# Attention loads in another order on the DMA queue, a term-by-term order for one matrix product, and weight halves split between its groups

## The reference

```python
def _attn_ref(q, k, v, beta):            # (4, 8, 768, 48)
    k_n = k / (np.linalg.norm(k, axis=-1, keepdims=True) + 1e-06)
    for t in range(S):
        kt, vt, bt = (k_n[:, :, t], v[:, :, t], beta[:, :, t, None])
        y[:, :, t] = np.einsum('bhd,bhde->bhe', q[:, :, t], state)
        v_old = np.einsum('bhde,bhd->bhe', state, kt)
        state = state + bt[:, :, :, None] * np.einsum('bhd,bhe->bhde', kt, vt - v_old)
...
def _moe_ref(x, w_ch1, w_ch2):           # x (4, 768, 384), w_ch1 (384, 1536), w_ch2 (1536, 384)
    X = np.fft.fft(x, axis=1)
    X = np.fft.fft(X, axis=2)
    u = x + np.real(X)
    un = (u - mu) / np.sqrt(var + 1e-06)
    return u + np.maximum(un @ w_ch1, 0.0) @ w_ch2
...
def _moe2_ref(x, w_in, w_spatial, b_spatial, w_out):   # the gated block, not changed
```

## Time and profile before

| | us |
|---|---|
| median of 3 runs | 889.29 |
| lowest, highest | 888.91, 891.04 |
| time of the profiled execution | 889.29 |
| its span, first to last instruction | 887.5 |
| PE busy | 822.8 |
| DVE busy | 473.3 |
| ACT busy | 294.3 |
| POOL busy | 197.8 |

### The profile page before, as it was taken

How to read it: one execution, slowest core, us unless ns; L and a number is a source line. 1 busy time by engine, 2 the same in 40 slices (tenths; PEclk the granted TensorE clock), 3 DMA queues, 4 the chain that set the end, 5 groups by cost and what they waited for, 6 DMA issues and landing times.

```text
span 887.5 us, 24710 instructions
## 1 busy us (share of the span) xinstructions
PE 822.8 (93%) x10634; PEld 797.0 (90%) x10634; DVE 473.3 (53%) x1072; ACT 294.3 (33%) x656; POOL 197.8 (22%) x171
## 2 busy tenths in 40 slices
PE   7378999899886999999999999999999999999998
PEld 6377899888776999999999999999899899899898
DVE  4999999999278743443434443333732431431421
ACT  5235566656343121112211221122531431421412
POOL 2123123034005605300720000000222222222321
PEclk9658989889996999999999999999999999999999
DMA  6544445412572120111002003003410010000001
GB/s 196 147 132 125 139 131 155 118 57 80 164 248 96 59 68 18 53 51 40 18 18 71 0 18 119 18 18 112 144 54 31 23 53 35 18 0 36 19 1 54
DMA packets 38170, 65.14 MB, mean 73 GB/s; under 512 B 4345, under 2 KB 26178, under 8 KB 38082
## 3 DMA queue, kind: packets, MB, share of 16 engines
q1 hardware_dynamic: 38082, 63.85, 23.2%
HBM read 46.66 MB, written 14.16 MB: 69 GB/s over the span
## 4 chain that ended last, share of the span: by engine, by line
PE 62%; issue 21%; DVE 13%; POOL 2%; ACT 2%; DMA 1%; SPq 0%; POOLq 0%; DVEq 0%; ACTq 0%
PE m_ps_h L1189 12%; PE g_ps_v L1690 11%; PE m_ps_d L1174 11%; PE ps_ga L449 4%; PE g_ps_y L1690 3%; PE g_ps_u L1690 3%; DVE prod L619 3%; PE ps_r L500 3%; DVE t_lane L623 2%; PE ps_y L540 2%; PE ps_y L535 2%; PE ps_u L518 2%; PE ps_s L553 2%; POOL g_vn_lo L1587 2%; PE ps_ga L474 2%
## 5 line engine op out<-in xcount | busy, mean ns | idle before, releaser
L1374 DVE SCALAR_TENSOR_TENSOR m_h_lo<-m_ps_h,m_h_hi 128x512 fp32r<-128x512 f32 x72 | 49.7, 691 | 101.7 <-ACT m_h_hi L1051 101.7
L1174 PE MATMUL m_ps_d<-m_w_hi,m_h_hi 128*128 128x384 f32 x288 | 97.6, 339 | 0.0
L1174 PE MATMUL m_ps_d<-m_w_hi,m_h_lo 128*128 128x384 f32 x288 | 96.3, 335 | 0.0
L1174 PE MATMUL m_ps_d<-m_w_lo,m_h_hi 128*128 128x384 f32 x288 | 96.3, 334 | 0.0
L1051 ACT ACTIVATE m_h_hi<-m_ps_h 128x512 fp32r<-128x512 f32 x72 | 43.1, 598 | 151.7 <-PE m_ps_h L1189 151.5
L449 PE MATMUL ps_ga<-kq 64*64 64x64 f32 x1536 | 61.0, 236 | 19.0 <-DVE t_lane L623 12.4
L1189 PE MATMUL m_ps_h<-m_unt_hi,m_w_hi 128*128 128x256 f32 x432 | 75.3, 283 | 3.4 <-DVE m_h_lo L1374 2.4
L449 PEld LDWEIGHTS ps_ga<-kq 64*64 64x64 f32 x1536 | 57.3, 150 | 19.9 <-DVE t_lane L623 12.6
L1189 PE MATMUL m_ps_h<-m_unt_hi,m_w_lo 128*128 128x256 f32 x432 | 74.3, 281 | 0.0
L1189 PE MATMUL m_ps_h<-m_unt_lo,m_w_hi 128*128 128x256 f32 x432 | 74.2, 281 | 0.0
L619 DVE TENSOR_TENSOR prod<-g_lane,t_lane 128x31 f32<-128x31 f32 (+15 forms) x186 | 69.6, 374 | 6.2
(11 more groups left out here) (223 smaller groups left out, 1920.7 us busy)
## 6 DMA issues: line engine op xcount, KB each, us to landing
kq<-kq_g SPq DMA_DIRECT2D x48, 256.0 KB, 3.3
v_in<-v_g SPq DMA_DIRECT2D x12, 384.0 KB, 3.3
k_in<-k_g SPq DMA_DIRECT2D x12, 384.0 KB, 3.1
x_scr<-y_sb SPq DMA_DIRECT2D x24, 192.0 KB, 3.5
stage<-w_ch SPq DMA_DIRECT2D x6, 768.0 KB, 5.7
x_scr<-m_x_sb SPq DMA_DIRECT2D x24, 192.0 KB, 1.9
g_x<-x_scr SPq DMA_DIRECT2D x24, 192.0 KB, 4.5
out<-g_y SPq DMA_DIRECT2D x24, 192.0 KB, 1.9
```

What stands on the lines that cost most here:

```text
L1174: last = pe.matmul(out, first[x], second[y], start=(k == 0 and m == 0), stop=(k == n - 1 and m == 2))
L1374: dve.scalar_tensor_tensor(h_lo[:, 2 * g:2 * g + 2].rearrange("p f t -> p (f t)"), ps_h[g % 2][:, :], 0.0, h_hi[:, 2 * g:2 * g + 2].rearra ...
```

## The change

Three edits, and no instruction is added or taken away on PE, DVE, ACT or POOL.

1. The SP list of the attention steps is written in another order. The wait on y_ok inside a step is gone. The last two quarters of a group's second kq half move from places 6 and 7 to places 0 and 1 of the next group, the second half of v from place 2 to place 1, and the store `results(g, 0)` ahead of the loads of place 7.
2. `hidden` waits for t_lo before its first product, and takes the 9 products of a tile through `three`: the three terms of one slice d after each other.
3. The low halves of chunks 3 and 4 move into the first `hidden`: DVE does chunk 3 after the group 0, chunk 4 after group 2, chunk 5 after group 4.

```diff
                 if k and k <= STEPS - NB:
                     sp.wait_ge(u_ok, k)
+                if n == N - 1 and g + 1 < G:
+                    results(g, 0)
                 if g and n < NB - 1:
                     results(g - 1, n + 1)
...
-                if 2 <= k <= STEPS - NB:
-                    sp.wait_ge(y_ok, k - 1)
...
+                if n < 2 and g + 2 < G:
+                    for p in ((2 + n,) if g else (2 * n, 2 * n + 1)):
+                        load_kq(g + 2, 1, p)
...
+                if 2 <= n < 6 and g + 3 < G:
+                    if g and n == 2:
+                        sp.wait_ge(y_done, N * g)
+                    load_kq(g + 3, 0, n - 2)
...
+                if n >= 6 and g + 3 < G:
+                    load_kq(g + 3, 1, n - 6)
...
-                pe.wait_ge(t_hi, b * R + (r + 1))
+                pe.wait_ge(t_lo, b * R + (r + 1))
...
-                            if f == 0 and m == 2:
-                                pe.wait_ge(t_lo, b * R + (r + 1))
...
+                        for d in range(DT):
+                            last = three(ps_h[g % 2][:, C2 * (f % 2):C2 * (f % 2) + C2],
...
-                    if first and g == 2:
-                        weights(WC - 1)
+                    if first and g % 2 == 0:
+                        weights(DT + g // 2)
...
-            weights(DT, NS)
             batch(0, True, False)
```

More of the change, by code:

```diff
@@ L221, in sync @@
                 g, n = k // N, k % N
-                two, three = g + 2 < G, g + 3 < G
                 if k and k <= STEPS - NB:
                     sp.wait_ge(u_ok, k)
+                if n == N - 1 and g + 1 < G:
+                    results(g, 0)
                 if g and n < NB - 1:
                     results(g - 1, n + 1)
-                if n == (1 if g else 0) and two:
+                if n == (1 if g else 0) and g + 2 < G:
                     diagonal(g + 2)
[L229 to L241, removed]
-                if 2 <= k <= STEPS - NB:
-                    sp.wait_ge(y_ok, k - 1)
-                if n in (0, 2) and g + 1 < G:
+                if n < 2 and g + 2 < G:
+                    for p in ((2 + n,) if g else (2 * n, 2 * n + 1)):
+                        load_kq(g + 2, 1, p)
+                if n < 2 and g + 1 < G:
                     if g and n == 0:
                         sp.wait_ge(preset_ok, p_count(N * g - 1) - 1)
-                    load_v(g + 1, n // 2)
+                    load_v(g + 1, n)
+                if 2 <= n < 6 and g + 3 < G:
+                    if g and n == 2:
+                        sp.wait_ge(y_done, N * g)
+                    load_kq(g + 3, 0, n - 2)
                 if n in (3, 5) and g + 1 < G:
@@ L1184, in hidden @@
                     for f in (2 * g, 2 * g + 1):
-                        for m, (w, t) in enumerate(((w1_hi, unt_hi), (w1_lo, unt_hi), (w1_hi, unt_lo))):
-                            if f == 0 and m == 2:
-                                pe.wait_ge(t_lo, b * R + (r + 1))
-                            for d in range(DT):
-                                last = pe.matmul(ps_h[g % 2][:, C2 * (f % 2):C2 * (f % 2) + C2],
-                                                 w[:, d, P * f:P * f + P], t[:, d], start=(m == 0 and d == 0),
-                                                 stop=(m == 2 and d == DT - 1))
+                        for d in range(DT):
+                            last = three(ps_h[g % 2][:, C2 * (f % 2):C2 * (f % 2) + C2],
+                                         [w[:, d, P * f:P * f + P] for w in (w1_hi, w1_lo)],
+                                         [t[:, d] for t in (unt_hi, unt_lo)], d, DT)
                     last.then_inc(h_done, 1)
```

## The result

| | before | after |
|---|---|---|
| runs on the same chip | 20 | 20 |
| median, us | 889.87 | 894.60 |
| lowest, highest | 885.21, 899.02 | 890.12, 901.16 |
| mean | 890.12 | 894.89 |
| profiled execution, us | 889.29 | 894.69 |

The forecast was 890.4, within 0.3% of no change. A second comparison of the same two kernels gave +4.1, give or take 1.1, so the loss is real. The single executions of one kernel scatter by about 3 us either way, and what follows has to live with that. The means count every run; in each series of the kernel before at most one run lies over 1.5% above its fastest and counts as slow, and without it the differences would be up to 0.5 us higher.

A forecast was written before the change was run, and what follows sets the result against it. PE was taken as the bound, by its own pace in the mixer and by instruction arrival in the attention. 889.29 + 0.7 (attention) + 0 (hidden pace) + 0.4 (first hidden) gave 890.4 us, range 886.6 to 895.0.

The forecast's parts named there:

- The first hidden: Mixer's first hidden: group 2 starts 0.9 us earlier, group 3 waits 2.4 us through POOL's port; +0.4 us at `result`.
- The bound and the stretches: Whole kernel: PE's own pace bounds the mixer after its first 26 us; the attention has 15.2 us of instruction-issue holes.
- The pace of the nine products: Hidden stages: term-by-term order leaves each at its pace, 113.3 or 117.8 ns a product; 0 us.
- The second rival: Hidden stages: term-by-term order may make all of them slow, +2.4 us, 892.8 us with the other terms; chance 0.12.
- the third: All hidden stages at 113.3 ns, 3.4 us less, or instruction packets relieved, 2.8 us less; 886.5 us, chance 0.12.
- Edit 1 as data: Attention: the removed waits guard no data and no load comes so late that PE must wait; costs nothing.
- Edit 1 as company of instruction packets: Attention: denser transfers in places 0 and 1 hold PE's instruction packets longer; +0.9 us, between 5.6 gained and 9 lost.
- the price of a meeting: Attention: an instruction packet beside heavy traffic holds its engine 1.86 instead of 0.99 us, at most 0.87 us more.
- Well over 19: Attention, 84 to 250 us: PE's issue waits should sum to 14 to 18 us; well over 19 would mean the first rival.
- the first rival: Attention: dense transfers in places 0 and 1 delay most instruction packets of the coupling products; 894 us, chance 0.20.
- The wait on t_lo: Start of hidden: PE starts 1.05 us later in the first one; 0 in the other 11.
- DVE caught again by POOL and its tokens late: Behind the first hidden: if POOL holds up both DVE operations again, tokens come 1.1 us later and the term is +1.2.

The follow-up runs named there:

- dense: The kernel before with all kq and k loads of a group at place 1, v loads at place 0, no y_ok wait: +2.4 ± 0.8 us, ratio 1.0040.
- calm: The kernel before with all kq, k and v loads of groups 1 to 3 at places 2 to 6, no y_ok wait: -2.5 ± 0.6 us, ratio 0.9983.
- the repeat: The whole change measured a second time against the kernel before: +4.1 ± 1.1 us, ratio 1.0048.
- null: The kernel before with the three slices d of hidden taken in falling order, all else the same: +0.2 ± 1.0 us, ratio 1.0016.
- the second look at edit 1: The SP list of the change alone, measured a second time against the kernel before: +2.4 ± 1.1 us, ratio 1.0030.
- few bytes: The kernel before, list and waits kept, with late kq loads cut to an eighth and k and v loads to a sixteenth: -6.3 ± 0.7 us, ratio 0.9938.

## Why the prediction was wrong, step by step

Two terms of the sum failed. The attention stood in it at +0.7 us and costs 1.5 ± 0.5 by the fit (1.2 by the direct comparison, 2.4 on top of edits 2 and 3). The first hidden stood in it at +0.4 and costs 1.7 to 1.8 us by the profiles, 2.1 to 2.6 by the timed kernels. In both the mechanism was named rightly and priced too low, and in both the prediction counted only the time that PE stands, not the lower clock that follows. The forecast change was +1.1 us, the measured one +4.8 and +4.1.

**The bound and the stretches: right.** PE is full behind 311 us, and the time from the second transposes to the end is the same in both kernels within 0.1 us.

**The pace of the nine products: right.** Term by term or slice by slice, 113.3 and 117.8 ns, each in the stages where it was before. The second rival (all stages slow) and the third (all fast) did not happen.

**Edit 1 as data: right.** No PE wait for kq, v or k in after, and taking only the y_ok wait away shows no cost (-1.1 ± 1.2).

**Edit 1 as company of instruction packets: right in mechanism, too small in size.** The step that failed is the price of a meeting, "at most 1.86 - 0.99 = 0.87 us". It charged a packet that is being moved beside other traffic, and took that as the whole harm. In after the packets are as long as before, and PE still stood for 2.49 us. PE goes on 1.1 to 1.65 us behind a packet's end, and in all six profiles with the changed list the packet starts 5.5 to 6.3 us behind the one before it, against 3.6 to 4.7: the loss lies before a packet starts. That this is a wait in the DMA queues behind the run of dense transfers is what the rows of 95 to 102 us suggest; no record shows when the packet was asked for, so it stays argued. What is shown is the dependence: with the same number of packets, 76 instead of 122 GB/s takes 6.3 us off, and the placement alone, dense against calm, both without the y_ok wait, is worth 4.9 us.

The second half of the same step is the clock. The prediction priced holes as time that PE stands, and a hole also leaves a stretch at the lower clock behind it. Each run lists its mean granted clock, and twice what it lacks to 1, times the span, is the time at the lower clock. Over 137 runs of the kernel before, the time rises by 0.27 us for each us of it (0.22 to 0.31 in the four series); this is what goes together and not yet a cause. The mean is 84 us in these runs, 97 us in 37 runs of the changed kernel and 91 us in its second comparison: by the slope 3.5 and 2.0 us of the 4.8 and 4.1. In the profile, after had 10 us more of it up to the last y copy, by the slope 2.8 us, while the sum of its holes rose by 0.6 us only. "Well over 19 is the first rival" was thus the wrong sign to look for: the sum was 15.8, inside of the forecast's 14 to 18, and this execution had lost 4.7 us there all the same; over six profiles it was 16.0, and the end of the attention 3.5 us later. In size the direct comparison gives 1.2 ± 0.75 for edit 1 against +0.7 predicted, and the comparison on top of edits 2 and 3 (4.5 for the change, 2.1 without edit 1) 2.4 ± 1.2.

**The wait on t_lo: right.** 1.05 us later in the first hidden, nothing in any other.

**The first hidden: the mechanism was right, the term was too small.** The port wait of DVE behind POOL, the loss of the wait at group 2 and the new one at group 3 all came: 2.44 and 2.61 us in two profiles where 2.4 was worked out, 1.11 and 1.38 in the other two with edits 2 and 3. One sum of the step does not come out of its own terms: 283.4 + 0.6 + 0.69 is 284.7 and not 285.05, but measured, h_lo of group 0 is there 5.57 us behind the first product, near the 5.65 that 285.05 stands for. Two things were missing from the term.

The larger is again the clock. A wait of 2.4 us was counted as 2.4 us. In the repeat and in the kernel with edits 2 and 3 on the calm list it left 3.4 us at the lower clock, 1.6 us more; the profiled before, which waited 1.96 us at group 2, kept the full clock from 282.6 us on. In the profile of after the wait was 1.11 us and no such stretch followed, but there the first hidden had begun at the lower clock and kept it until 289.4, 5.4 us, where before it was 4.2.

The other is that the sum was made against one profile. Its 1.96 us at group 2 is the longest wait there of the eight profiles with neither edit 2 nor edit 3; the others have 1.68, 1.31, 1.25, 1.13 and three times 0. In these three (dense, null, and the second look at edit 1) DVE's second subtraction slipped in ahead of POOL and took 1.75 us instead of 5.0. So there was on the mean less to win at group 2 than the prediction set against its new wait.

From the last y copy to the second transposes the four profiles with edits 2 and 3 take 44.9 us on the mean (44.1 to 45.5), and the eight with neither 43.1 us (42.2 to 44.2): +1.7, where the term was +0.4. Counted from the first transposes to the second, where nothing ahead of the edited stage comes in, it is 30.6 against 28.8 us: +1.8 ± 0.4, with 29.3 for edit 2 and 29.4 for edit 3 alone (three profiles each). The profile of edit 2 alone has the longest way of all 18 from the last y copy to the second transposes, 46.8 us, but 16.3 of them lie ahead of its first transposes, where the others have 14.1 to 15.0. What the prediction kept as a case, DVE caught again by POOL and its tokens late, is in the row at 310.41 us: 1.09 us where it was 0.28.

**The sum.** By the profiles' segment +1.7 for edits 2 and 3, by the timed kernels 2.1 ± 1.0 and 2.6 ± 1.1; by the direct comparison and the fit another 1.2 to 1.5 for edit 1. That makes 3 to 4 of the 4.4 us. The rest, about 1 us, is inside the errors and has no owner. The prediction's first rival, 894 by delayed packets, comes nearest in its number, but about half of that is the first hidden's.

**What stays open.** How the loss divides between edits 1 and 3: edit 3 by the fit costs 2.3 us, but its three profiles without edit 2 take 43.5 us for the segment, 0.4 above the eight. One of the three lost another 1.6 us behind the second transposes, the other two nothing, and no profile shows where the rest could lie. Whether edits 1 and 3 cost more together than apart (4.5 against 1.2 + 1.2, each ± 1) cannot be told at a scatter of 3 us. Why one wait of PE is followed by the lower clock and another is not is open too.

## What to carry to other kernels

Traffic that nobody waits for can still be on the critical path of a long unrolled stage, through the instruction packets of the busiest engine; keep it away from the steps with the most instructions (4.9 us between dense and calm here), and price a wait of PE with the lower clock that it may leave behind, which added two thirds to it in two profiles here. When a term rests on a wait in one profile, ask what sets its length, since one that happens to be long promises more than can be won on the mean. And before a sum of terms of 0.3 to 1 us is believed, note how far executions of the same kernel scatter: here two profiles of the same kernel put the end of the attention 5.4 us apart.

## What the runs showed of the hardware

- Cutting data traffic in the attention from 122 to 76 GB/s (windows from 84 to 250 us) made the kernel 6.3 ± 0.7 us faster with as many instruction packets (41 against 40) of the same length; PE's holes fell from 15.2 to 10.1 us.
- 334 of 339 stops of PE over 0.15 us between 84 and 250 us, in 18 profiles, end 1.1 to 1.65 us behind the end of an instruction packet. With the changed list the packet behind that of 95 to 96 us starts 5.5 to 6.3 us after it in six profiles, with the list of before 3.6 to 4.7 us in five.
- The length of an instruction packet does not show its harm: 1.1 to 1.2 us on the mean in before, after, dense, calm and few bytes alike.
- Two PE waits at group 3 of the first hidden, of 2.44 and 2.61 us, were followed by 3.4 us at the lower clock each; waits of 1.11 and 1.38 us at the same group were not, nor was one of 1.96 us at group 2 before, but neither was one of 2.93 us at group 2 in the profile of edit 2 alone. What decides is open. In the calm kernel with edit 3 a stretch at the lower clock began behind a wait of 2.29 us at the second transposes, and it is the one profile of 18 that took 584.1 us from them to the end instead of 582.5; waits of 2.38 and 2.37 us at the same place in the profiles of edit 3 and of edits 1 and 3 had none behind them.
- A DVE subtraction with both inputs in SBUF takes 1.75 us alone and, started just after a POOL operation of 3.5 us, 3.8 to 5.1 us; in the two profiles of the change the POOL operation ahead of it kept its length (3.50 and 3.51 us).
- Which of the two paces, 113.3 or 117.8 ns for 256 columns at the full clock, a stage has does not depend on the order of its nine products.
